# An attention and two dense layers in one kernel: the opening and the last two tiles put in another order

## The reference, cut to what matters

```python
# q, k, v: (4, 8, 768, 64); per head a decaying state, token by token
state = gamma * state + outer(k[t], v[t])
y[t] = scale * q[t] @ state
x = y as (3072 tokens, 512)
# first dense layer, 512 -> 2048 -> 512
h = x @ w_in
g = where(h >= 1, h, where(h <= -1, 0, (h + 1)**2 / 4))
x = g @ w_out
# second dense layer, 512 -> 1024 -> 512
h = x @ w_in2
solu = h * softmax(h)
ln = (solu - mean) / sqrt(var + 1e-6) * g_ln
out = ln @ w_out2
```

## Time and profile before

| | |
|---|---|
| median of 3 runs | 885.4 us (884.4 to 888.78) |
| device time of the profiled execution | 884.47 us |
| its span | 882.6 us |
| PE busy | 868.1 us, 98% of the span |
| DVE, ACT, POOL busy | 401.7, 282.8, 204.8 us |
| bytes moved | 82.83 MB, 94 GB/s over the span |

### The profile page before, as it was taken

How to read it: one execution, slowest core, us unless ns; L and a number is a source line. 1 busy time by engine, 2 the same in 40 slices (tenths; PEclk the granted TensorE clock), 3 DMA queues, 4 the chain that set the end, 5 groups by cost and what they waited for, 6 DMA issues and landing times.

```text
span 882.6 us, 11875 instructions
## 1 busy us (share of the span) xinstructions
PE 868.1 (98%) x4864; PEld 710.8 (81%) x4864; DVE 401.7 (46%) x645; ACT 282.8 (32%) x438; POOL 204.8 (23%) x185
## 2 busy tenths in 40 slices
PE   6999999999999999999999999999999999999997
PEld 5788888888888888888878888888888888888886
DVE  4444443333433243333433333443666666666662
ACT  2333342122212132221321232334344444444432
POOL 2555433223222323222212122226000000000000
PEclk9999999999999999999999999999999999999999
DMA  9912102111111112211111004300444444444442
GB/s 347 344 49 71 62 12 86 48 48 48 51 58 48 48 36 80 64 49 37 48 36 48 25 1 167 120 1 0 144 136 159 148 143 143 155 144 162 148 139 100
DMA packets 50741, 82.83 MB, mean 94 GB/s; under 512 B 5248, under 2 KB 23680, under 8 KB 50688
## 3 DMA queue, kind: packets, MB, share of 16 engines
q1 hardware_dynamic: 50400, 81.56, 27.3%
q10 hardware_dynamic: 288, 0.53, 0.2%
HBM read 56.90 MB, written 25.17 MB: 93 GB/s over the span
## 4 chain that ended last, share of the span: by engine, by line
PE 96%; DMA 1%; SPq 1%; DVE 0%; ACT 0%; issue 0%; DVEq 0%
PE acc L360 31%; PE h L347 29%; PE o_ps L731 15%; PE h L716 15%; PE att L281 2%; PE att L292 2%; PE att L316 1%; DMA mask<-in_mask 1%; PE att L306 1%; SPq L194 1%; SPq L211 0%; SPq L212 0%; ACT w L387 0%; DVE w L511 0%; ACT g_raw L436 0%
## 5 line engine op out<-in xcount | busy, mean ns | idle before, releaser
L360 PE MATMUL acc<-g_hi,w 128*128 128x512 f32 x768 | 257.1, 396 | 0.0
L347 PE MATMUL h<-x_hi,w 128*128 128x512 f32 x768 | 252.3, 389 | 3.2 <-DVE x_lo L476 2.1
L624 POOL TENSOR_TENSOR g_lo<-g_raw,g_hi 128x512 fp32r<-128x512 f32 x96 | 123.4, 1286 | 403.0 <-ACT g_hi L387 403.0
L436 ACT ACTIVATE g_raw<-g_raw,half_bias 128x512 f32<-128x512 f32 x96 | 69.6, 724 | 341.9 <-DVE g_raw L560 341.9
L360 PEld LDWEIGHTS acc<-g_hi,w 128*128 128x128 f32 x768 | 144.1, 188 | 35.1 <-issue 3.4
L347 PEld LDWEIGHTS h<-x_hi,w 128*128 128x128 f32 x768 | 144.1, 188 | 33.5 <-ACT x_hi L387 2.4
L360 PE MATMUL acc<-g_lo,w 128*128 128x512 f32 x384 | 149.6, 390 | 0.0
L347 PE MATMUL h<-x_lo,w 128*128 128x512 f32 x384 | 149.4, 389 | 0.0
L560 DVE TENSOR_SCALAR g_raw<-h 128x512 f32<-128x512 f32 x96 | 66.2, 690 | 178.5 <-PE acc L360 177.8
L565 DVE TENSOR_TENSOR g_raw<-h,g_raw 128x512 f32<-128x512 f32 x96 | 66.4, 692 | 70.0 <-ACT g_raw L436 70.0
L347 PEld LDWEIGHTS h<-x_lo,w 128*128 128x128 f32 x384 | 72.1, 188 | 14.9
(11 more groups left out here) (68 smaller groups left out, 814.5 us busy)
## 6 DMA issues: line engine op xcount, KB each, us to landing
z<-zq SPq DMA_DIRECT2D x24, 512.0 KB, 2.6
zt<-z SPq DMA_DIRECT2D x96, 128.0 KB, 2.9
kT<-in_kT SPq DMA_DIRECT2D x24, 256.0 KB, 2.6
q<-in_q SPq DMA_DIRECT2D x24, 256.0 KB, 2.7
v<-in_v SPq DMA_DIRECT2D x24, 256.0 KB, 3.0
x2T<-y SPq DMA_DIRECT2D x24, 256.0 KB, 2.5
x_raw<-x2T SPq DMA_DIRECT2D x12, 512.0 KB, 4.4
out<-o SPq DMA_DIRECT2D x24, 256.0 KB, 2.0
```

The costliest lines, as they stand in the source:

```text
L347: last = mm(hb[f % 2][:, :], ww, xx[:, kt, :], start=kt == 0 and t == 0, stop=kt == KT - 1 and t == 2)
L360: last = mm(acc[m][:, :], ww, gg[:, f % 2, :], start=f == 0 and t == 0, stop=f == FT1 - 1 and t == 2)
L436: nc.scalar.activation(gate[:, f % 2, :], gate[:, f % 2, :], ACT.Square, bias=half_bias[:, 0:1], scale=0.5).then_inc(sem["squared"], 1)
L624: tt(g[1][:, f % 2, :], gate[:, f % 2, :], g[0][:, f % 2, :].bitcast(F32), ALU.subtract)\
```

## The change

What it does, engine by engine:

- **SP** now loads `first_mask` itself, behind kT and q of chunks 0 and 1. w_in and w_out are loaded apart: w_in of slices 0 to 2 ahead of `tables`, w_in 3 among the kn, w_out 0 behind them; `g_ln` moves behind chunk 4.
- **PE** makes three matmuls of 128x256 on a zeroed tile (`warm_up`) ahead of everything, and three more behind the scores of chunk 1. `up(0, 0)` becomes `first_up`: two halves of 256 columns, each as four high-by-high matmuls, four with the low weights, four with the low activations, with a wait in front of each group; the half for chunks 0 and 1 does not wait for chunks 2 and 3. The first updates move two slots later (`FIRST_UPDATE`).
- **ACT** splits w_in and w_out in two instructions, w_in of slices 0 to 2 ahead of the dense work and each w_out in the step of its slice. **POOL** makes the low part of w_in 0 ahead of the scaling of kn, and each w_out's low part behind `g_lo` of its slice. **DVE** waits for `mask`, `tables` and `g_ln` where it first uses them.
- In the second layer the last two `up` stand ahead of the last five `down`, and on DVE and ACT the steps of tiles 22 and 23 are interleaved.

```diff
-W_READY = 2
+W_READY = 3
+WARM_UP = 3
+FIRST_UPDATE = 2
...
@@ -220,25 +225,36 @@
-            for c in range(2):
+                if c == 1:
+                    sp.dma_start(mem["first_mask"][:, :, :, :].rearrange("p e a t -> p (e a t)"), io["first_mask"])\
+                        .then_inc(sem["first_mask"], 16)
+            for c in range(B):
                 load("v", c)
-            load_weights(0)
-            for c in range(2, B):
-                load("v", c)
-            load_weights(1)
+                if c == 1:
+                    load_w_in(0)
+            for f in range(1, W_READY):
+                load_w_in(f)
             sp.dma_start(tables[:, :], io["tables"]).then_inc(sem["tables"], 16)
             for c in range(B):
                 load("kn", c)
-            load_weights(2)
+                if c == 1:
+                    load_w_in(W_READY)
+            load_w_out(0)
+            load_w_in(W_READY + 1)
+            load_w_out(1)
...
-            for f in range(3, FIRST_PIECE):
-                load_weights(f)
+            sp.dma_start(mem["g_ln"][:, :], io["g_ln_col"]).then_inc(sem["gains"], 16)
+            for f in range(2, FIRST_PIECE):
+                if f + W_READY < FIRST_PIECE:
+                    load_w_in(f + W_READY)
+                load_w_out(f)
...
             def attention(j, slot):
-                if j == 1 and slot < B:
-                    update(slot)
+                if j == 1 and 0 <= slot - FIRST_UPDATE < B:
+                    update(slot - FIRST_UPDATE)
                 for c, stage in at_slot(j, slot, STAGES):
...
-                if n == 0:
-                    pe.wait_ge(sem["x0_hi"], B)
-                    pe.wait_ge(sem["x0_lo"], B)
                 wait(pe, sem["gmax"], n - 1)
                 if blk == 0:
-                    wait(pe, sem["w_in_lo"], f + 1)
+                    wait(pe, sem["w_in_lo"], f)
...
+            def first_up():
+
+                for b in (0, 2):
+                    xs = slice(b * P, (b + 2) * P)
+                    pe.wait_ge(sem["x0_hi"], b + 2)
+                    if b == 0:
+                        pe.wait_ge(sem["w_in_hi"], 1)
+                    for t, (wn, xn) in enumerate(((0, 0), (1, 0), (0, 1))):
+                        if t == 1:
+                            pe.wait_ge(sem["w0_in_lo"], 1)
+                        if t == 2:
+                            pe.wait_ge(sem["x0_lo"], b + 2)
+                        for kt in range(KT):
+                            last = mm(hb[0][:, xs], w[0][:, wn, kt * P:(kt + 1) * P], x[xn][:, kt, xs],
+                                      start=t == 0 and kt == 0, stop=t == 2 and kt == KT - 1)
                 last.then_inc(sem["h_ready"], 1)
...
-            for c in range(B):
+            def warm_up():
+                for n in range(WARM_UP):
+                    mm(acc[KT - 1][:, 0:2 * P], mem["warm"][:, 0:P], mem["warm"][:, :], start=True, stop=True)
+
+            pe.wait_ge(sem["warm"], 1)
+            warm_up()
+            scores(0)
+            scores(1)
+            warm_up()
+            for c in range(2, B):
                 scores(c)
             for c in range(B):
                 outputs(c)
...
-                        split_weights(f + W_READY)
+                    if blk == 0:
+                        if f + W_READY < FT1:
+                            split_w_in(f + W_READY)
+                        split_w_out(f)
...
-            act.dma_start(mem["first_mask"][:, :, :, :].rearrange("p e a t -> p (e a t)"), io["first_mask"])\
-                .then_inc(sem["first_mask"], 16)
-            act.dma_start(mem["g_ln"][:, :], io["g_ln_col"]).then_inc(sem["gains"], 16)
             act.wait_ge(sem["half_set"], 1)
-            nc.scalar.activation(mem["warm"][:, :], half_bias[:, :], ACT.Copy)
-            for c in range(B - 1):
+            nc.scalar.activation(mem["scratch"][:, :], half_bias[:, :], ACT.Copy)
+            first_split(0)
+            split_w_in(0)
+            for c in range(1, B):
                 first_split(c)
-            split_weights(0)
-            first_split(B - 1)
             for f in range(1, W_READY):
-                split_weights(f)
+                split_w_in(f)
...
                 mask_scores(c)
-            for c in range(B - 1):
+            for c in range(B):
                 first_split(c)
-            split_weights(0)
-            first_split(B - 1)
             for f in range(1, W_READY):
                 split_weights(f)
-            dve.wait_ge(sem["tables"], 16)
-            dve.wait_ge(sem["mask_loaded"], 16)
-            dve.wait_ge(sem["gains"], 16)
...
-                    if blk == 0 and f + W_READY < FT1:
-                        split_weights(f + W_READY)
+                    if blk == 0:
+                        split_weights(f)
...
-            for f in range(W_READY):
-                split_weights(f)
+            pool.wait_ge(sem["w_in_hi"], 1)
+            tt(w[0][:, 1, :], w_raw[0][:, 1, :], w[0][:, 0, :].bitcast(F32), ALU.subtract)\
+                .then_inc(sem["w0_in_lo"], 1)
...
-                if t >= LAG2:
+                if LAG2 <= t < TILES - 2:
                     down(t - LAG2)
-            for t in range(TILES - LAG2, TILES):
+            for t in range(TILES - 2 - LAG2, TILES):
                 down(t)
...
+            for t in range(TILES - 2):
+                if t >= 2 and t % 2 == 0 and t // 2 + 1 < TILES // 2:
+                exponential(t)
+                squares(t)
                 if t == 0:
                     finish["act_evacuate"]()
                 if t >= LAG2:
                     output(t - LAG2)
                 if t:
                     split_z(t - 1)
-            output(TILES - 3)
+            exponential(TILES - 2)
+            squares(TILES - 2)
+            exponential(TILES - 1)
+            split_z(TILES - 3)
+            squares(TILES - 1)
+            output(TILES - 5)
+            split_z(TILES - 2)
+            output(TILES - 4)
             split_z(TILES - 1)
-            output(TILES - 2)
-            output(TILES - 1)
+            for t in range(TILES - 3, TILES):
+                output(t)
...
+            for t in range(TILES - 2):
+                if t >= 2 and t % 2 == 0 and t // 2 + 1 < TILES // 2:
+                    split_x(t // 2 + 1)
+                maximum(t)
+                softened(t)
+                if t == 0:
+                    finish["dve_evacuate"]()
+                normalized(t)
                 if t:
                     split_z(t - 1)
+            maximum(TILES - 2)
+            softened(TILES - 2)
+            maximum(TILES - 1)
+            normalized(TILES - 2)
+            softened(TILES - 1)
+            split_z(TILES - 3)
+            normalized(TILES - 1)
+            split_z(TILES - 2)
             split_z(TILES - 1)
```

More of the change, by code:

```diff
@@ L93, in place @@
     plain("half_bias", [P, 1])
-    plain("warm", [P, 1])
+    plain("scratch", [P, 1])
+    plain("warm", [P, BLK // 2])
     for name in STATISTICS:
@@ L348, in up @@
                                   stop=kt == KT - 1 and t == 2)
+                last.then_inc(sem["h_ready"], 1)
+            def first_up():
[12 more added lines that the diff above has]
+                                      start=t == 0 and kt == 0, stop=t == 2 and kt == KT - 1)
                 last.then_inc(sem["h_ready"], 1)
@@ L365, in dense @@
                 for f in range(FT1):
-                    up(blk, f)
+                    if blk == 0 and f == 0:
+                        first_up()
+                    else:
+                        up(blk, f)
                     if blk < BLOCKS - 1:
@@ L481, in take_outputs @@
                 dve.wait_ge(sem["y_ready"], c + 1)
+                if c == B:
+                    dve.wait_ge(sem["tables"], 16)
                 if b == 0:
@@ L503, in attention @@
             def attention(j, slot):
-                if j == 1 and slot < B:
-                    add_update(slot)
+                if j == 1 and 0 <= slot - FIRST_UPDATE < B:
+                    add_update(slot - FIRST_UPDATE)
                 for c, stage in at_slot(j, slot, STAGES):
@@ L569, in dense @@
                         prepare(f)
+            nc.vector.memset(mem["warm"][:, :], 0.0).then_inc(sem["warm"], 1)
             nc.vector.memset(half_bias[:, :], 0.5).then_inc(sem["half_set"], 1)
@@ L764, in output, with exponential @@
                 copy(o[:, t % 2, :], op[t % 2][:, :]).then_inc(sem["o_ready"], 1)
-            for t in range(TILES):
-                if t >= 2 and t % 2 == 0 and t // 2 + 1 < TILES // 2:
-                    split_x(t // 2 + 1)
+            def exponential(t):
                 act.wait_ge(sem["neg_max"], t + 1)
@@ L802, in split_z, with maximum @@
                         .then_inc(sem["zT_lo"], 1)
-            dve.wait_ge(sem["power_set"], 1)
-            for t in range(TILES):
-                if t >= 2 and t % 2 == 0 and t // 2 + 1 < TILES // 2:
-                    split_x(t // 2 + 1)
```

(7 more changed lines are left out.)

32 lines of the change are left out of this document (21 added, 11 removed).

## The result

In seven runs each, the changed kernel took **880.19 us** (median, 879.24 to 880.74) and the kernel before 885.2 us (884.06 to 888.78): a ratio of 0.9942, 95% interval 0.9929 to 0.9955. The profiled execution took 879.7 us (before: 884.47), its span is 877.6 us (before: 882.6).

What follows compares the result with a forecast made beforehand. PE bounds the kernel; only its waits at both ends can shrink. Gains of 4.8 (opening) and 1.8 (last tiles), 6.6 us, give 877.9 from the profiled 884.47, or 878.8 from the 885.4 median; range 876.8 to 881.6.

Steps and rivals of the forecast that it cites:

- The first loads: Opening: first mask moved behind q1 lets q0 land at 4.8 us; q2 and q3 as before, 8.85 and 10.2 us.
- Warm-up and scores: Opening scores on PE: chunk 0 still slow, chunk 1 nearly fast, second group costs 0.4 us; outputs from 11.7 us.
- The first product: `first_up` in halves of 256 columns: 0.125 us a matmul, 3.0 us, from 15.4 to 18.4 us, later splits covered.
- The rule of the Trainium skill: Rival for `first_up`: each matmul also pays its load, one after the other, 7.2 us; 883.0 us, chance 0.04.
- Loads as the pace: Rival for `first_up`: loads set the pace of the halves, 4.5 us; 880.3 us, chance 0.08.
- From there to the first `down`: From `first_up` to the end of `down(0)`: 10.9 us, ending at 29.3 instead of 34.07 us; opening gain 4.8 us.
- Behind the opening: Slices after the opening: ACT's second copy a slice and POOL's moved splits lie hidden behind PE, costing nothing.
- The last tiles: End of the second layer: earlier `up(23)` removes PE's wait for `zT_lo` before the last `down`; gain 1.8 us, or 0.
- The rival of the second group in the way: Opening: PE still slow at chunk 1 and in the group, chunk 2 starts 2.2 us later; 881.0 us, chance 0.10.
- The other rivals: POOL last 879.8 (0.08); transfers pace opening 883.6 (0.03); loads pace 880.3 (0.08); load then matmul 883.0 (0.04); 256-column price 889.7 (0.03).

Runs made afterwards that it cites:

- experiment 3: Changed kernel with `first_mask` issued from ACT's queue at the start again, as before the change: 881.22 us, ratio 0.9956.
- experiment 8: Changed kernel with DVE waiting for `tables`, `mask` and `g_ln` ahead of the dense work again, loads in their new order: 887.85 us, ratio 1.0034.
- experiment 5: The changed kernel again, unedited, as a control: 880.17 us, ratio 0.9951.
- Experiment 2: Changed kernel with the first product in whole rows of 512 columns again, behind all four chunks: 881.14 us, ratio 0.9958.
- experiment 4: Changed kernel with w_out splits drawn forward, two a slice in slices 7 to 9, none in 13 to 15: 879.54 us, ratio 0.9938.
- experiment 11: Changed kernel with w_out splits two a slice in slices 7 to 9, none in 13 to 15, and the four first q on ACT's queue: 878.3 us.
- experiment 12: Changed kernel with w_out splits two a slice in slices 7 to 9, none in 13 to 15, measured once more: 880.41 us, ratio 0.995.
- Experiment 7: Changed kernel with the last tiles of the second layer in the old order: 881.33 us, ratio 0.9966.
- experiment 10: Changed kernel with the four q of the opening issued from ACT's queue, all else as changed: 880.34 us, ratio 0.9949.
- experiment 6: Changed kernel without the second group of warm-up matmuls, the first kept: 880.86 us, ratio 0.9953.
- experiment 1: Changed kernel without both groups of warm-up matmuls: 881.17 us, ratio 0.9961.

## Why the prediction was right, and where not

The forecast was 878.8 us with a range to 881.6; the time is 880.19. Of 6.6 us expected in the span, 5.0 came. Of the 1.6 that are missing, 0.3 are the opening's, 0.2 the slow restart of the `up` behind it (2.94 us instead of 2.72), 0.8 the end of block 0 and 0.2 the start of the second layer. The step that failed is in the sentence "ACT's second copy a slice and POOL's moved splits lie in the same step, hidden behind PE".

- **The first loads**: q0 was said to land at 4.8 us; it was there by 4.19, without a wait. Right in direction, and experiment 3 shows why: with the mask beside it, 5.90. But "q2 and q3 land as before" was wrong. One queue alone moved 252 and 346 GB/s from 4 to 8 us, and chunks 2 and 3 started at 9.44 and 10.77 us, both on q. In other executions with this opening chunk 2 started at 9.1 (experiment 8) to 11.6 us (experiment 5).
- **Warm-up and scores**: the first scores were to stay slow, 2.08 us; they took 1.29. Over the executions with an early q0 the first group took between 1.16 and 2.08 us, so my assumption was one end of it. The second group took 1.56 us (1.3 assumed), ended at 8.85 and cost nothing here, because q was later. These errors cancel: outputs at 11.86 us against 11.7 forecast, 15.57 against 15.4 at their end.
- **The first product**: 0.128 us a matmul against 0.125 assumed, 3.07 us against 3.0, with no wait. The rule of the Trainium skill that stood against it (page "TensorE: Matmul & The Clock Gate", Part 3, The mechanism: a weight load overlaps matmuls in flight only if it uses other row groups) would have made it 7.2 us; the trace disagrees at 256 columns as it did at 512. The same section also lets a load into the "background weight buffer" go ahead of matmuls in flight, which the prediction left out; no run here shows where these loads went. Loads as the pace, 4.5 us, are out as well: the 0.188 us of a load's bar is no lower bound for the distance of two matmuls. Experiment 2 shows the cover that the halves give: 1.47 us.
- **From there to the first `down`**: 10.9 us forecast, 29.59 - 18.64 = 10.95 measured. POOL was ready at 24.84 us, before PE at 25.96, with 1.1 us to spare instead of 0.4. Here too errors cancel: scaling kn took 4.99 us, not 4.04, since the first two of the four lay beside DVE's low parts of w_in and took 1.54 and 1.49 us instead of 1.04, but it began 0.8 us sooner than said, and `g_lo` took 1.28 us, not 1.75. Gain of the opening 4.48 against 4.8; the difference is the 0.17 us of the outputs, 0.07 of `first_up` and 0.05 here. Experiment 8 shows the part that removing DVE's waits plays: with them the new order of loads would lose to the old one.
- **Behind the opening**: forecast 0, measured -0.8 us at the end of block 0 and -0.2 at the second layer's start. In the steady slices the moved splits are hidden, as said. But that of slice 14, which before ran two slices earlier, now falls on the one step in which ACT, DVE and POOL have the next block's activations to split, and there PE begins 1.25 us behind DVE's first low part (114.96 less 113.71) instead of 1.77 (119.21 less 117.44). So ACT's copy takes 0.52 us of lead. POOL's low part takes 0.59 more: DVE's second low part ends 2.56 us behind the start of the first (116.27 less 113.71) instead of 1.97. In the kernel before, PE had 0.48 us to spare there; 1.11 us are more than that. That the splits are the cause is shown: the three profiles in which they are moved away (experiments 4, 11 and 12) have no such wait. The parts of ACT and POOL are read from the rows; no experiment took them apart. The 0.2 us at the second layer's start are no work of the splits: they go with the load of `x_raw`. It took 3.86 us in the kernel before and 3.84 in experiment 4, where nothing was lost, 4.11 in the changed kernel and in experiment 11, where 0.2 us were, and 4.59 in experiment 12, where 0.7 were. Why it varies was not found.
- **The last tiles**: 1.8 us forecast, 1.76 measured. `zT_hi` was to start at 868.6 us by the time of the kernel before; less the 3.24 us by which PE is ahead there, that is 865.4, and it started at 865.27. The last transpose was to end at 864.96 - 3.6 = 861.4, so 858.1, and ended at 858.18. The low parts were done at 867.22, 1.6 us before PE came (2 said). So this term came out by its own steps, not only in size. Experiment 7 gives the term back: a wait of 1.6 us, 1.2 us by the medians.

The rival of the second group in the way (881.0 us) is not what happened in the first profile. Experiments 5 and 12 show executions in which it did, PE being slow at chunk 1 and in the group (2.04 and 2.29 us, 2.08 and 2.33); in experiment 3 the group was fast but late. The other rivals did not occur.

Two things stay open. Why q and kT of the opening land up to 2 us apart in executions of the same instructions was not found. And whether two queues help the opening isn't settled: experiment 10 was no faster than the control, and what experiment 11 had in its opening may be the luck of the landing.

## What to carry to other kernels

When work is moved later by a fixed number of steps, look at the last steps it lands in, not at the steady ones: there it may meet work that comes once a block. A wait on a load belongs at the load's first use; put ahead of a loop, it holds everything behind it on that engine, and an idle TensorE can then pay a second time at the lower clock. Of an opening that hangs on loads, compare several executions before a microsecond is given to an edit.

## What the runs showed of the hardware

- The granted clock fell from 1.00 to 0.50, 2.4 to 1.2 GHz, after PE had stood 1.85 us early in experiment 5, and during its 6.53 us in experiment 8; after a stand of 1.51 us in experiment 6 the scores kept 1.16 us. In experiment 1 the row says 1.00 from 4 to 14 us while the scores take 2.08 us instead of 1.16: the row doesn't show the first rise after the start.
- Three float32 matmuls of 128x256 (6 instructions) took 1.56 us at the fast pace and 2.93 at the start, so 0.52 and 0.98 each; with rounded operands a matmul of that size took 0.128 us.
- DVE's low parts of a w_in slice or of `y`, whose inputs both lie in SBUF, took 0.68 us alone. Those that began while a POOL instruction ran ended about 0.55 us behind its end: at 22.29, 27.32, 32.48 and 114.48 us of the changed kernel they took 1.40, 1.37, 1.36 and 1.78 us, and POOL ended at 23.14, 28.14, 33.29 and 115.72. POOL's low parts beside these took 1.73 to 1.76 us instead of 1.28. The low parts of the attention's outputs, which DVE reads from PSUM, kept 0.69 us beside POOL (at 14.63 us, POOL at work from 14.19 to 15.47). What the two contend for was not tried.
